# Six attention groups: scores times values and state products joined in one TensorE slot, ScalarE's steps in slots of their own

## The chip, the cores and the metric

One core of one Trainium2 chip runs the whole program. The metric is device time in microseconds from start to end of one execution, median of the runs. Engines are PE (TensorE; PEld is its weight load), DVE (VectorE), ACT (ScalarE), POOL (GpSimd) and SP (SyncE, which issues the DMAs).

## What is computed

The reference chains three parts, all in float32. Batch is 4, sequence 768.

```python
# attention with a decaying state, 8 heads of size 48
state = alpha[:, :, t, :, None] * state + einsum('bhd,bhe->bhde', k[:, :, t], v[:, :, t])
y[:, :, t] = einsum('bhd,bhde->bhe', q[:, :, t], state)
# x = y with its heads side by side: (4, 768, 384)
h = x.transpose(0, 2, 1) @ U @ V                 # token mixing of rank 32
u = x + h.transpose(0, 2, 1)
x = u + maximum(u @ w_ch1, 0) @ w_ch2            # 384 -> 1536 -> 384
h = maximum(x @ w_in, 0); u, v = halves(h)       # gated block, 384 -> 1024
x = (u * (w_spatial @ normed(v) + b_spatial)) @ w_out
```

## The kernel before

The attention of one batch is done in two groups of four heads. A group's sequence is cut into chunks of 128 positions. Inside a chunk the decayed scores are built in eight levels (steps 0 to 7); step 8 (`T_STEP`) transposes the keys, step 9 (`KV_STEP`) forms key-value products whose running sums are the states, steps 10 to 12 multiply scores with values (one for each of three PSUM banks `YB[y]`, L867), and step 13 (`Y_STEP`, L876) adds queries times states into the same three banks.

The attention of batch 0 runs first, alone. After it, a loop over the batches on every engine walks through a fixed list `UNITS1` of the first feed-forward's work: one token-mixing unit ("xu"), six transposing units ("u"), then 24 "h" units (`up`, L885) and 24 "z" units (`down`, L962 to L964), alternating with a lag of two. An "h" or "z" unit is nine matmuls of 128x384. Ahead of each unit every engine does the attention steps of batch b+1 that the table `SLOTS[b]` puts there. So for three batches, two groups each, six groups are woven in. A slot is the place ahead of one unit; a step's place in a group is `POSITION[n]`, a fraction of the group's half of the batch, and `step_slots` turns it into a unit by the units' estimated times. Engines follow their own instruction order and meet at semaphores only.

Which engine does what at a step (functions `att_step` on PE and ACT, `att_piece` on DVE):

- Steps 10 to 12: only PE works (the matmuls of L867, 32 for each step). `AV_STEP` is 10.
- Step 10 is also `START_STEP`: ACT copies the first two spreads of the next group's queries (L1045, four copies) with `att_start` and `att_second`, and DVE forms the next group's decay totals (L1338).
- Step 12 (`Y_STEP - 1`): ACT copies the states to `St` (L1138), two copies.
- Step 13: PE does L876 for all three banks, waiting for `state_ready` and for the last `q_ready`; ACT copies the three banks to `xn` (L1152); DVE scales the next group's queries (`PREFIX_STEP`, L1372 and L1374).

On PE step 10 waits for the copies of the scores (`a_act`, `ad_copied`), step 12 for the state sums of DVE (`state_step`), since its bank held the key-value products. With this table the four steps of a group have four slots in a row, between units that alternate "z", "h", "z", "h"; only in the first woven batch, second group, do steps 12 and 13 share one.

The two hidden-layer buffers of PSUM (`HB`) are emptied by ACT (L1190) and DVE (L1514): `up` of unit f waits for unit f-2's low parts, `down` of unit f for unit f's own, which is two "h" units back. SP's loads, the state sums of DVE and POOL's scaling (L655) are in the same order as the steps 0 to 9 need them. After the last batch's units the gated block runs by itself for all four batches.

Of the kernel before, what the change touches and what calls it, by code (L numbers as in the profile page):

```python
# [14 lines left out]
BATCH, HEADS, SEQ, HD = 4, 8, 768, 48  # L15
# [32 lines left out]
T_STEP, KV_STEP, AV_STEP = LEVELS, LEVELS + 1, LEVELS + 2  # L48
Y_STEP = AV_STEP + YB
STEPS = Y_STEP + 1  # L50

START_STEP, PREFIX_STEP = AV_STEP, Y_STEP
START, PREFIX = -1, -2


# [118 lines left out]
def step_slots(lead):  # L174

    ends = np.cumsum([time for _, _, time in UNITS1])
    slots = [[] for _ in UNITS1]
    for g in range(GROUPS):
        for n in range(STEPS):
            at = lead + (1 - lead) * (g + POSITION[n]) * SPREAD / GROUPS  # L180
            slots[int(np.searchsorted(ends, at * ends[-1]))].append((g, n))
    return slots


def vector_slots(slots):

    out, waiting = [], []
    for j, unit in enumerate(UNITS1):
        now = []
        for g, n in slots[j]:  # L190
            now += waiting
            waiting = [(g, n, piece) for piece in range(vector_pieces(n))]
            now += waiting
            waiting = []
            if n == START_STEP:
                now.append((g, START, 0))
            if n == PREFIX_STEP:
                now.append((g, PREFIX, 0))
        if not slots[j]:
            now += waiting[:1]  # L200
            waiting = waiting[1:]
        out.append(now)
    assert not waiting
    return out


def vector_pieces(n):

    return 2 if n < MASKED else NKV if n == KV_STEP else int(n < LEVELS)
# [1 line left out]


SPREAD = 0.96
POSITION = [(0.5 + 8.8 * n / KV_STEP) / 12 for n in range(AV_STEP)] + [x / 12 for x in (9.9, 10.4, 10.9, 11.4)]
ARENA = 212800
LEAD = [0.07] + [0.0] * (BATCH - 2)
SLOTS = [step_slots(lead) for lead in LEAD]
# [11 lines left out]
def build(nc, q, k, al, v, u_w, v_w, w1, w2, win, wst, wout, bias, ident_d, mask_d, out):  # L229
# [3 lines left out]
    with ExitStack() as ctx:  # L233
# [214 lines left out]
        def cut(src, hi, lo, n):  # L448
            flat = [x.rearrange("p a b -> p (a b)") for x in (src, hi[:, :, :], lo[:, :, :])]
            return [tuple(x[:, i * PIECE:(i + 1) * PIECE] for x in flat) for i in range(n)]  # L450

        first = cut(w1, w1h, w1l, W1_PIECES)
# [304 lines left out]
        def _(pe):  # L757
# [262 lines left out]
            for b in range(BATCH):  # L1020
                for j, (kind, i, _) in enumerate(UNITS1):
                    if b < BATCH - 1:
                        for g, n in SLOTS[b][j]:
                            att_step(b + 1, g, n, False)
                    if kind == "xu":
                        token_mix(b)
                    elif kind == "u":
                        mixed(b, i)
                    elif kind == "h":
                        up(b, i)  # L1030
                    else:
                        down(b, i)
# [7 lines left out]
        def _(act):  # L1040
# [53 lines left out]
            def att_step(a, g, n, first):  # L1094
                w = space(a, g)
                pa, pg = before(a, g)
                if 1 <= n < MASKED - 1:

                    act.wait_ge(q_ready[g], (LEVELS - 1) * a + n)
                    act.wait_ge(score_done[g], SCORES * a + n)  # L1100
                    spread(a, g, n + 1, False)
                if n == LEVELS - 2:

                    if first:
                        act.wait_ge(zeroed_a[g], 1)
                    else:

                        act.wait_ge(aux_done[pg], AUX * pa + AUX)
                    act.wait_ge(score_done[g], SCORES * a + n + 1)
                    L = block_size(n)  # L1110
                    for hh in range(2):
                        for m in range(2):
                            o = HALF * m + BLOCK * hh
                            bank = score_bank(w, n)[o:o + L, 0:UNITS * L].rearrange("p (u t) -> p u t", t=L)
                            dst = w.A[2 * L * m:2 * L * m + L, :, hh, 2 * L * m + L:2 * L * (m + 1)]
                            last = nc.scalar.copy(dst, bank)
                    last.then_inc(a_act[g], 1)
                if n == LEVELS - 1:

                    for p in range(PAIRS):  # L1120
                        act.wait_ge(score_done[g], SCORES * a + n + p + 1)
                        for hh in range(2):
                            bank = score_bank(w, n, p)[hh * HALF:(hh + 1) * HALF, 0:NCH * HALF]
                            last = nc.scalar.copy(w.A[0:HALF, p * NCH:(p + 1) * NCH, hh, HALF:CH],
                                                  bank.rearrange("p (u t) -> p u t", t=HALF))
                        last.then_inc(a_act[g], 1)
                if n == KV_STEP and not first:
                    square_copies(a, g, QUARTERS)
                if n == Y_STEP - 1:

                    if first:
                        act.wait_ge(zeroed_a[g], 2)
                    else:
                        act.wait_ge(aux_done[pg], AUX * pa + AUX)
                    act.wait_ge(state_step[g], NKV * (a + 1))
                    for hh in range(2):
                        r, e = slice(hh * ROW1, hh * ROW1 + HD), slice(hh * HD, (hh + 1) * HD)
                        last = nc.scalar.copy(w.St[r, :, :, e], w.Sc[r, :, :, :])  # L1138
                    last.then_inc(state_ready[g], 1)
                if n == T_STEP and not (first and g == 0):  # L1140
                    for x, units in enumerate(T_BANKS):
                        act.wait_ge(aux_done[g], AUX * a + x + 1)
                        nc.scalar.copy(w.kT[:, units[0]:units[-1] + 1, :],
                                       w.TB[x][:, 0:len(units) * ROWS].rearrange("p (u r) -> p u r", r=ROWS)
                                       ).then_inc(aux_act[g], 1)
                if n == Y_STEP:
                    if not first:

                        act.wait_ge(u_done, NU * a)
                    for y in range(YB):  # L1150
                        act.wait_ge(aux_done[g], AUX * a + AUX_KV + y + 1)
                        nc.scalar.copy(xn[:, 2 * y:2 * y + 2, g * GW:(g + 1) * GW],  # L1152
                                       w.YB[y][:, 0:2 * GW].rearrange("p (m x) -> p m x", m=2)
                                       ).then_inc(aux_act[g], 1)
# [115 lines left out]
            for b in range(BATCH - 1):  # L1270
                for j, (kind, i, _) in enumerate(UNITS1):
                    for g, n in SLOTS[b][j]:
                        att_step(b + 1, g, n, False)
                        if b == g == 0 and n in SPLITS2:
                            split_high(SPLITS2[n])
                        na, ng = after(b + 1, g)
                        if n == START_STEP and na < BATCH:
                            att_start(na, ng, False)
                            att_second(na, ng)
                    high(b, kind, i)  # L1280
                    if b == 0 and (kind, i) == ("u", NU - 1):
                        att_start(1, 0, False)
                        att_second(1, 0)
# [30 lines left out]
        def _(dve):  # L1314
# [354 lines left out]
            for b in range(BATCH):  # L1669
                for j, (kind, i, _) in enumerate(UNITS1):  # L1670
                    if b < BATCH - 1:
                        for g, n, piece in VECTOR_SLOTS[b][j]:
                            na, ng = after(b + 1, g)
                            if n == START and na < BATCH:
                                att_start(na, ng)
                            elif n == PREFIX and na < BATCH:
                                att_prefix(na, ng)
                            elif n >= 0:
                                if b == g == n == piece == 0:
                                    att_prefix(1, 0)  # L1680
                                att_piece(b + 1, g, n, piece, False)
                    low(b, kind, i)
                    if b == 0 and (kind, i) == ("u", NU - 1):
                        att_start(1, 0)
                    if b == BATCH - 1 and kind == "h" and i in COMBINES:
                        combine(COMBINES.index(i))
# [47 lines left out]
```

## Time and profile before

| what | us |
|---|---|
| median of 3 runs | 739.6 |
| lowest, highest run | 738.36, 743.63 |
| the profiled execution's own time | 741.86 |
| its span, first to last instruction | 740.1 |

The profile is of one execution. Each engine's row gives the time it was busy, its share of the span and its instructions. In a timeline a row is a run of like instructions in order: start, time to the end of the last, engine, line, tile written and read, count, and in brackets the idle time ahead and what ended it. Each matmul call of 32-bit floats of L867 and L876 appears as two MATMUL records, with two LDWEIGHTS records; the calls of L885 and L962 to L964 as one.

### The profile page before, as it was taken

How to read it: one execution, taken by the hardware profiler on the slowest of the kernel's cores; microseconds unless marked ns; L12 is line 12 of the kernel's file. 1: busy time of each engine (PE TensorE's matmuls, PEld its weight loads, DVE VectorE, ACT ScalarE, POOL GpSimd, SP SyncE). 2: the span in 40 equal slices, each digit the busy share in tenths (PEclk: the TensorE clock that was granted, in tenths of full speed). 3: DMA queues.
4: the chain of work that ended last, by engine and by line, in shares of the span. 5: the costliest groups of instructions: out<-in, count | busy, mean ns of one | idle time of the engine just before them, and what ended most of it. 6: DMA issues, size and time to landing. Idle time of an engine off the chain costs nothing.

```text
span 740.1 us, 25675 instructions
## 1 busy us (share of the span) xinstructions
PE 703.6 (95%) x11336; PEld 664.0 (90%) x11336; DVE 395.9 (53%) x668; ACT 338.4 (46%) x573; POOL 210.5 (28%) x141
## 2 busy tenths in 40 slices
PE   2798899999999999999999999999999999999998
PEld 2688789899998899999999899999998998999998
DVE  6888674544664555555553324225933851870671
ACT  5787546435546346446435331334433432532422
POOL 5504480320350220161120231462360060033022
PEclk9999999999999999999999999999999999999999
DMA  9414501211401221311000251002110101101001
GB/s 360 157 46 148 176 4 45 99 57 45 152 4 45 73 83 45 118 37 45 22 18 2 91 150 72 33 11 87 64 40 26 65 12 53 64 0 64 0 0 64
DMA packets 16525, 49.49 MB, mean 67 GB/s; under 512 B 1616, under 2 KB 9552, under 8 KB 15920
## 3 DMA queue, kind: packets, MB, share of 16 engines
q1 hardware_dynamic: 16432, 48.09, 18.5%
q8 instruction: 77, 1.26, 0.7%
q14 instruction: 16, 0.13, 0.1%
HBM read 38.65 MB, written 9.44 MB: 65 GB/s over the span
## 4 chain that ended last, share of the span: by engine, by line
PE 67%; issue 19%; POOL 4%; DVE 3%; ACT 1%; DMA 0%; POOLq 0%; DVEq 0%; ACTq 0%
PE HB L885 23%; PE ZB L962 7%; PE ZB L964 7%; PE ZB L963 7%; PE SB L762 4%; PE ZB L885 3%; PE SB L885 3%; POOL gl L712 3%; PE SB L867 2%; PE SB L876 2%; PE SB L822 2%; POOL x2l L686 1%; PE SB L999 1%; PE SB L837 1%; PE SB L850 1%
## 5 line engine op out<-in xcount | busy, mean ns | idle before, releaser
L1514 DVE SCALAR_TENSOR_TENSOR hid_lo<-HB,hid_hi 128x384 fp32r<-128x384 f32 x96 | 53.3, 556 | 140.9 <-ACT hid_hi L1190 140.1
L1190 ACT ACTIVATE hid_hi<-HB 128x384 fp32r<-128x384 f32 x96 | 47.2, 492 | 158.9 <-PE HB L885 158.7
L885 PE MATMUL HB<-uh,w1h 128*128 128x384 f32 x288 | 103.0, 358 | 4.1 <-DVE ul L1510 1.5
L962 PE MATMUL ZB<-hid_hi,w2h 128*128 128x384 f32 x288 | 98.6, 342 | 0.0
L885 PE MATMUL HB<-ul,w1h 128*128 128x384 f32 x288 | 96.7, 336 | 0.0
L964 PE MATMUL ZB<-hid_lo,w2h 128*128 128x384 f32 x288 | 96.6, 335 | 0.0
L885 PE MATMUL HB<-uh,w1l 128*128 128x384 f32 x288 | 96.5, 335 | 0.0
L963 PE MATMUL ZB<-hid_hi,w2l 128*128 128x384 f32 x288 | 96.3, 334 | 0.0
L1045 ACT COPY Qd<-Q 48x768 f32<-48x768 f32 x84 | 73.0, 870 | 13.6 <-PE SB L762 5.0
L712 POOL TENSOR_TENSOR gl<-gf,gh 128x384 fp32r<-128x384 f32 x32 | 33.2, 1044 | 147.8 <-ACT gh L1230 147.4
L655 POOL TENSOR_TENSOR Q<-Q,bk 112x768 f32<-112x768 f32 x13 | 24.7, 1902 | 174.4 <-ACT Qd L1045 174.4
L762 PEld LDWEIGHTS SB<-Qd,K 112*32 112x32 f32 x4032 | 42.1, 116 | 25.4 <-issue 16.8
L762 PE MATMUL SB<-Qd,K 112*32 112x32 f32 x4032 | 46.9, 205 | 16.1 <-DMA K<-in_k 9.3
L655 POOL TENSOR_TENSOR Q<-Q,small 112x768 f32<-112x768 f32 x26 | 42.0, 1617 | 67.8 <-PE SB L810 31.3
L885 PEld LDWEIGHTS HB<-uh,w1h 128*128 128x128 f32 x288 | 54.0, 187 | 6.6 <-issue 1.4
L1331 DVE TENSOR_TENSOR K<-K,small 112x768 f32<-112x768 f32 x26 | 47.7, 1834 | 16.8 <-PE SB L822 9.5
L1606 DVE BATCH_NORM_STATS2 stats<-vf 128x6 f32<-128x512 f32 x24 | 16.5, 692 | 73.1 <-ACT vf L1234 73.1
L885 PEld LDWEIGHTS HB<-uh,w1l 128*128 128x128 f32 x288 | 54.2, 188 | 1.3 <-issue 1.3
L962 PEld LDWEIGHTS ZB<-hid_hi,w2h 128*128 128x128 f32 x288 | 54.0, 188 | 1.1
L885 PEld LDWEIGHTS HB<-ul,w1h 128*128 128x128 f32 x288 | 54.0, 188 | 0.2 <-issue 0.2
L963 PEld LDWEIGHTS ZB<-hid_hi,w2l 128*128 128x128 f32 x288 | 54.1, 188 | 0.0
L964 PEld LDWEIGHTS ZB<-hid_lo,w2h 128*128 128x128 f32 x288 | 54.1, 188 | 0.0
(260 smaller groups left out, 1516.4 us busy)
## 6 DMA issues: line engine op xcount, KB each, us to landing
Q<-in_q SPq DMA_DIRECT2D x8, 768.0 KB, 6.0
AL<-in_al SPq DMA_DIRECT2D x7, 768.0 KB, 4.9
K<-in_k SPq DMA_DIRECT2D x7, 768.0 KB, 4.3
Vt<-in_v SPq DMA_DIRECT2D x8, 576.0 KB, 3.9
mid<-x2s SPq DMA_DIRECT2D x8, 576.0 KB, 3.6
x<-mid SPq DMA_DIRECT2D x4, 1152.0 KB, 5.3
out<-o_sb SPq DMA_DIRECT2D x24, 192.0 KB, 1.8
x2s<-in_w SPq DMA_DIRECT2D x9, 384.0 KB, 4.6
```

The costliest lines, as they stand in the source:

```text
L655: nc.gpsimd.tensor_tensor(qq, qq, t.broadcast_to([ROWS, FLAT // (2 * L), L]), ALU.mult).then_inc(q_ready[g], 1)
L712: nc.gpsimd.tensor_tensor(gl[:, f, t], gf[:, f, t], gh[:, f, t].bitcast(F32), ALU.subtract).then_inc(gl_done, 1)
L762: last = nc.tensor.matmul(bank[j * BLOCK:(j + 1) * BLOCK, u * BLOCK:(u + 1) * BLOCK], keys[:, first_key:first_key + BLOCK], queries[:, u, ...
L885: last = nc.tensor.matmul(dst, weights(x, w), moving(y, m), start=(n == 0 and x == y == 0), stop=(n == total - 1 and y == 1))
L962: nc.tensor.matmul(bank, w2h[:, i, cols], hi, start=(i == 0), stop=False)
L963: nc.tensor.matmul(bank, w2l[:, i, cols], hi, start=False, stop=False)
L964: nc.tensor.matmul(bank, w2h[:, i, cols], lo, start=False, stop=(i == F1B - 1)).then_inc(z_done, 1)
L1045: nc.scalar.copy(space(a, g).Qd[0 if first else n % 2][r, :, hh, :].rearrange("p u (n l) -> p u n l", l=block_size(n)), targets(Q[g][r, :] ...
L1190: nc.scalar.activation(hid_hi[:, i % HID, :], HB[i % 2][:, 0:TILE], ACT.Relu).then_inc(h_hi, 1)
L1331: nc.vector.tensor_tensor(kk, kk, t.broadcast_to([ROWS, FLAT // (2 * L), L]), ALU.mult).then_inc(k_ready[g], 1)
L1514: nc.vector.scalar_tensor_tensor(hid_lo[:, i % HID, :], HB[i % 2][:, 0:TILE], 0.0, hid_hi[:, i % HID, :].bitcast(F32), ALU.max, ALU.subtra ...
L1606: nc.vector.bn_stats(stats[:, i, :], vf[:, i, :]).then_inc(stat_done, 1)
```

## The change

The table of positions gets two more entries, numbers 14 and 15, that are no steps of PE or DVE but slots for ACT: `SPREADS_SLOT` at 9.9/12, where step 10 stood, and `STATES_SLOT` at 10.8/12, near where step 12 stood. Steps 10 to 13 all go to 11.3/12, which is the unit where step 13 stood. Steps are now put into slots in order of position. PE skips numbers 14 and 15.

By the table, steps 10, 11 and 12 of a group move from units 24, 25 and 26 to unit 27, and from 48, 49 and 50 to 51 (first woven batch: from 26, 27, 28 to 29, and from 49, 50 to 51). The order of instructions on DVE, POOL and SP is the same as before; on ACT too, except that in the first woven batch the second group's state copies come one unit earlier. Batch 0's attention is not touched.

```diff
-START_STEP, PREFIX_STEP = AV_STEP, Y_STEP
+PREFIX_STEP = Y_STEP
+SPREADS_SLOT, STATES_SLOT = STEPS, STEPS + 1
...
     for g in range(GROUPS):
-        for n in range(STEPS):
+        for n in sorted(range(len(POSITION)), key=lambda n: POSITION[n]):
             at = lead + (1 - lead) * (g + POSITION[n]) * SPREAD / GROUPS
...
-            if n == START_STEP:
+            if n == SPREADS_SLOT:
                 now.append((g, START, 0))
...
-POSITION = [(0.5 + 8.8 * n / KV_STEP) / 12 for n in range(AV_STEP)] + [x / 12 for x in (9.9, 10.4, 10.9, 11.4)]
+POSITION = [(0.5 + 8.8 * n / KV_STEP) / 12 for n in range(AV_STEP)] + [x / 12 for x in (11.3, 11.3, 11.3, 11.3, 9.9, 10.8)]
...
                         for g, n in SLOTS[b][j]:
-                            att_step(b + 1, g, n, False)
+                            if n < STEPS:
+                                att_step(b + 1, g, n, False)
...
-                if n == Y_STEP - 1:
+                if n == (Y_STEP - 1 if first else STATES_SLOT):
...
-                        if n == START_STEP and na < BATCH:
+                        if n == SPREADS_SLOT and na < BATCH:
                             att_start(na, ng, False)
                             att_second(na, ng)
...
-                            elif n >= 0:
+                            elif 0 <= n < STEPS:
```

## Rows read from the trace of the kernel before

**Rows 1.** Page: busy time of each engine; the chain that ended last, by engine
```profile
PE 703.6 (95%) x11336; PEld 664.0 (90%) x11336; DVE 395.9 (53%) x668; ACT 338.4 (46%) x573; POOL 210.5 (28%) x141
...
PE 67%; issue 19%; POOL 4%; DVE 3%; ACT 1%; DMA 0%; POOLq 0%; DVEq 0%; ACTq 0%
```

**Rows 2.** Timeline of PE, one group's steps 10 to 13 in their four slots
```profile
229.03 0.33 PE L885 MATMUL HB<-uh,w1l 128*128 128x384 f32 x1
229.20 0.34 PE L885 MATMUL HB<-ul,w1h 128*128 128x384 f32 x1
229.47 0.89 PE L867 MATMUL SB<-Vt,A 128*32 128x48 f32 x64
230.28 0.44 PE L962 MATMUL ZB<-hid_hi,w2h 128*128 128x384 f32 x1
230.56 0.33 PE L963 MATMUL ZB<-hid_hi,w2l 128*128 128x384 f32 x1
...
232.07 0.72 PE L867 MATMUL SB<-Vt,A 128*32 128x48 f32 x48
233.09 0.38 PE L867 MATMUL SB<-Vt,A 128*32 128x48 f32 x16 [0.30 <-issue]
233.39 0.44 PE L885 MATMUL HB<-uh,w1h 128*128 128x384 f32 x1
...
237.51 0.34 PE L964 MATMUL ZB<-hid_lo,w2h 128*128 128x384 f32 x1
237.78 1.86 PE L876 MATMUL SB<-St,Q 112*32 112x96 f32 x80
239.57 0.44 PE L885 MATMUL HB<-uh,w1h 128*128 128x384 f32 x1
239.85 0.34 PE L885 MATMUL HB<-uh,w1l 128*128 128x384 f32 x1
```

**Rows 3.** Timeline of PE, the group whose steps 12 and 13 share a slot
```profile
176.51 0.34 PE L964 MATMUL ZB<-hid_lo,w2h 128*128 128x384 f32 x1
176.77 0.89 PE L867 MATMUL SB<-Vt,A 128*32 128x48 f32 x64
177.48 1.84 PE L876 MATMUL SB<-St,Q 112*32 112x96 f32 x80
179.25 0.45 PE L885 MATMUL HB<-uh,w1h 128*128 128x384 f32 x1
179.54 0.34 PE L885 MATMUL HB<-uh,w1l 128*128 128x384 f32 x1
```

**Rows 4.** Timeline of ACT beside the slots of rows 2
```profile
230.09 3.70 ACT L1045 COPY Qd<-Q 48x768 f32<-48x768 f32 x4
235.29 0.49 ACT L1190 ACTIVATE hid_hi<-HB 128x384 fp32r<-128x384 f32 x1 [1.50 <-PE HB L885]
235.80 1.20 ACT L1138 COPY St<-Sc 48x480 f32<-48x480 f32 x2
```

**Rows 5.** DMA queue q8 and busy times, 90 to 411; busy times between two stalls
```profile
q8 instruction: 57, 0.93, 1.2%
...
90.00:411.00 321.00, 316.98 (x7216) 292.97 (x7215) 170.45 (x279) 161.69 (x273) 85.42 (x55) 1.00 0.15 52
...
192.27:233.07 40.80, 40.50 (x885) 37.41 (x885) 23.29 (x38) 22.55 (x37) 18.47 (x12) 1.00 0.17 57
```

**Rows 6.** A stall of PE; queue q8 in windows 149.1:150.2 and 152.8:153.9
```profile
150.30 0.56 PE L762 MATMUL SB<-Qd,K 112*32 112x32 f32 x41
151.52 0.47 PE L762 MATMUL SB<-Qd,K 112*32 112x32 f32 x34 [0.65 <-issue]
...
q8 instruction: 1, 0.02, 5.8%
...
q8 instruction: 1, 0.02, 5.5%
```

**Rows 7.** Busy times of the shortest 256 instructions of PE without a stall
```profile
92.81:95.73 2.92, 2.92 (x131) 2.63 (x134) 2.01 (x3) 2.81 (x4) 2.44 (x2) 1.00 0.03 8
```

## The prediction

> **What bounds the kernel now.** I read the page first: PE is busy for 703.6 of 740.1 us, DVE and ACT for about half of it, and the chain that ended last lies on PE and on its own issue for 86% [rows 1]. From 90 to 411 us, where the six woven groups run, PE is busy for 316.98 of 321.00 us [rows 5]. So in this stretch time is what PE's instruction order costs: what another engine does counts only where PE comes to wait for it. The second view is the timeline of PE around one group's steps 10 to 13 [rows 2]. It shows three things: how long a slot of small matmuls keeps the large ones away, that there is extra time at both of its edges, and one gap of PE inside a slot that no other engine ended ("issue"). The third view, queue q8, says what that gap is [rows 5, 6].
>
> **The switches that go.** Large matmuls start 0.17 us apart (229.03, 229.20) [rows 2]. The slot of step 10 lies between the starts 229.20 and 230.56: 1.36 us, less the two steps of 0.17 that would be there anyhow, is 1.01. Inside it 64 records start in 0.89 - 0.21 = 0.68 us, 10.8 ns apart (0.21 is the last record's own length, 233.09 to 233.47 less its 15 steps), so about 0.33 us of the slot is no matmul at all: 0.10 us on entering, 0.13 us after the last one, 0.10 us after the first large one. Step 13 alone takes 239.85 - 237.51 - 0.35 = 1.99 us [rows 2]. Where steps 12 and 13 share a slot, both take 179.54 - 176.51 - 0.35 = 2.68 us [rows 3]. Separate they cost 1.01 + 1.99 = 3.00, so one slot fewer saves 0.32 us. This is the kernel's own example of the change, and I take its price. Five groups have four slots each, which become one (three fewer each, 15); the group that already shares one loses two. 17 x 0.32 = 5.4 us saved. For the unseen join of step 10 to 11 the bounds are 0.29 (all but a quarter change of 0.05) and 0.33 us, which moves the sum by 0.3 at most.
>
> **What the joined slot adds: instruction fetch.** Every matmul is two instructions here, weights and product. PE ran 14431 of them from 90 to 411, and queue q8 moved 57 packets, 0.93 MB, in that time [rows 5]: one packet of 16 KB for each 253 recorded instructions, 256 with those of registers and semaphores that are not counted. The same number stands between stalls: from the one ending at 192.27 to the one ending at 233.07 PE and PEld have 885 + 885 = 1770 instructions, 1792 = 7 x 256 with 22 uncounted ones [rows 5]. So PE's stream comes in pages of 256, and such gaps stand on page borders. How late a page can be is seen at 150.30 to 151.52 [rows 6]. PE stops in the middle of a run of step 3's matmuls; the only q8 packet near starts and ends within 149.1 to 150.2 and takes 5.8% of 16 x 1.1 us, 1.0 us; PE goes on at 151.52, at least 1.3 and about 1.4 us after it landed. The next packet lies within 152.8 to 153.9, so it started 1.3 us after PE had entered the new page. I read this as: the next page is asked for on entering the present one, and can be run 1.3 + 1.0 + 1.4 = 3.7 us later. Before, that is nearly always hidden, since between two slots of small matmuls lie 9 or 18 large ones at 0.17 us.
>
> The joined slot is 3 x 64 + 80 = 272 products, 544 instructions, on end. Wherever it starts, it holds one whole page. A page of step 10 to 12 matmuls alone lasts 128 x 10.8 ns = 1.4 us; one that is half step 13 (80 records in 1.86 - 0.25 = 1.6 us, 20 ns each) lasts 2.0. Counting on from the border at 233.09 (which assumes that the stream's length ahead of each group stays), borders fall 9, 62, 188, 205, 76 and 93 instructions into the six slots, so four slots hold a page of the short sort and two a mixed one (196 and 179 instructions of it short, 1.7 us): 1.5 us as a mean. PE's sequencer runs ahead of the array by a queue that no row shows; I give it 0.6 us, and its bounds are 0 and 1. The stall is then 3.7 - 1.5 - 0.6 = 1.6 us in each group, 6 x 1.6 = 9.6 us. Bounds: 256 instructions passed without a stall in 2.92 us [rows 7], so the wait may be as short as that: 2.9 - 1.5 = 1.4, 8.4 us in all. From below nothing excludes zero, if that page was only luckily placed and more than one is held ready. From above, a page can come later than 3.7: the page ahead of the stall of rows 6 held 18 large matmuls (3.1 us) and parts of two slots, some 4.4 us of work, and PE still waited. Stalls of twice the size, 3.1 us, would give 18.6. I take 9.6, nearest to the one fetch that the rows show whole.
>
> The 0.5 us stall ahead of 233.09 (48 records take 0.72 with the last one's 0.21, so the next was due at 232.59) [rows 2] sits in a slot that goes; stalls of that sort will fall elsewhere by chance, and half of it, 0.2, is counted as gained, which rounding swallows.
>
> The Trainium skill, page "Runtime: NRT & Kernel Launch", section "Instruction fetch mechanics", says that instructions come in blocks of 16 KiB (256), the next one while the present is run, which the 57 packets bear out. The same section gives PE's buffer as 2048 instructions and says that issue is slower than the filling, so that a border's cost is mostly hidden; by that no stall would come in 544 instructions, and the sum would be -5.4 alone. The gap at 151.52 speaks against it.
>
> **The cover that goes.** ACT's four spreads (3.70 us from 230.09) ran beside the slots of steps 10 and 11, and its state copies (1.20 us) beside step 12 [rows 4]. Now large matmuls alone lie beside them. With unit "h" 9 ending at time 0 (229.47), PE does a "z", an "h" and a "z" unit, 9 x 0.173 = 1.56 us each, and enters the joined slot at 4.7. ACT is done with the spreads at 4.3, with the next hidden half (0.49) at 4.8 and with the states at 6.0; step 13 can start at 4.7 + 0.3 + 2.1 = 7.1 without any stall. "z" unit 10, which needs that hidden half, comes only after the joined slot. So 1.1 us stay over and I cost the moves on ACT at nothing. Step 12's wait for the state sums was met before the first slot, and DVE's, POOL's and SP's order stays; the K load of the next group is issued ahead of these slots. After the joined slot the copies to `xn` come at the same place as before. If the spreads began over 1.1 us late, step 13 would pay the rest.
>
> **Sum.** Against the profiled execution, 741.9 (span 740.1 and 1.8 around it): -5.4 + 9.6 - 0.2 = +4.0, so 745.9. That execution stands 2.3 us above the median of 739.6; for the median I forecast 739.6 + 4.0 = 743.6, rounded to 743.5. A measurement of this kernel can tell about 1% (7.4 us) from no change, so this is no change that can be told, on the slow side.
>
> **Rivals.**
> - Fetch keeps up (a second page is held ready, or the queue's lead covers the rest): only the switches count, 739.6 - 5.4 = 734. For it: a shared slot of 144 products had no stall [rows 3], and a page in 2.92 us had none [rows 7]. Against it: 144 products need not hold a whole page, and the stalls at 151.52 and 233.09 are there [rows 2, 6]. Chance 0.25.
> - Late fetches decide, the case that is clearly slower: the packet in a joined slot starts late, as the one in rows 6 must have, because other transfers or pages stand before it, and some slots pay twice (the first group's third border falls inside its slot). Each group then pays about 3 us: 18 - 5 = +13, 752. It decides from 2.2 us a stall upward (13 less 5.4 is over 7.4 us). For it: the page of rows 6 was such a fetch. Against it: no load of SP is issued near the joined slots. Chance 0.12.
> - The lost cover: the spreads or state copies finish late and step 13 waits for `state_ready`. Their 1.2 us behind the hidden half, in all six groups, would cost up to 7 us beside the -5.4: 741. The margin of 1.1 us speaks against it [rows 4], and in a stall it is hidden. Chance 0.08.
>
> **How the numbers follow.** The forecast has 0.55. Its own range is 740 to 747 (stalls of 1.0 to 2.1 us). Leaving out half of the late case and the edge of the first, the range is 733.5 to 749. Faster by over 1% (under 732.2) needs more than all switches, 0.05; slower by over 1% (over 747.0) is the late case and a little of the forecast's upper end, 0.14; within 1% is the rest, 0.81.
>
> **What would show it.** Right: one slot a group on PE with 192 records of L867 and 80 of L876, at 10.8 and 20 ns, and in each a gap of 1 to 2 us ended by "issue", a q8 packet landing about 1.4 us before its end; idle time of PE by issue up by some 9 us; step 13 never ended by ACT. Wrong: joined slots of about 4.0 us without a gap (0.3 + 2.1 + 1.6), which is the first rival; gaps ended by ACT L1138, which is the third; or a slot pace slower than 10.8 ns because the sequencer cannot feed 544 instructions so quickly, which no row here excludes beyond 144 products.

## The result and the profile after

| | median | lowest to highest |
|---|---|---|
| before, runs beside | 738.98 us | 738.21 to 743.63 |
| changed | 745.08 us | 743.03 to 745.44 |
| ratio, 95% interval | 1.0068 | 1.0043 to 1.0093 |

The changed kernel is 0.7% slower, clear of no change by its interval, and less than the 1% that the chances were drawn at. The forecast was 743.5 us. In microseconds the ratio is 5.0 of 739 (3.2 to 6.9); the two medians lie 6.1 apart, inside that interval.

The page of the changed kernel hardly shows where the time went. PE is busy for less time over a longer span, with the same number of instructions as in rows 1:

```profile
span 741.2 us, 25675 instructions
PE 696.9 (94%) x11336; PEld 662.1 (89%) x11336; DVE 395.5 (53%) x668; ACT 338.3 (46%) x573; POOL 210.6 (28%) x141
```

The waits of PE from 90 to 416 us (engine, tile and line, what ended the idle time: total, times, longest) name the place. L868 and L877 are what L867 and L876 were:

```profile
PE SB L868 <- issue: 5.3, 3, 1.9
PE SB L877 <- issue: 3.7, 3, 1.4
PE SB L763 <- issue: 0.9, 2, 0.6
PE SB L823 <- issue: 0.4, 1, 0.4
```

Six idle times, one for each woven group, none ended by another engine. The timeline of PE at the third group's joined slot, which answers to rows 2:

```profile
233.71 0.34 PE L965 MATMUL ZB<-hid_lo,w2h 128*128 128x384 f32 x1
233.98 2.25 PE L868 MATMUL SB<-Vt,A 128*32 128x48 f32 x192
236.04 0.84 PE L877 MATMUL SB<-St,Q 112*32 112x96 f32 x29
237.98 1.35 PE L877 MATMUL SB<-St,Q 112*32 112x96 f32 x51 [1.09 <-issue]
239.25 0.44 PE L886 MATMUL HB<-uh,w1h 128*128 128x384 f32 x1
239.53 0.34 PE L886 MATMUL HB<-uh,w1l 128*128 128x384 f32 x1
```

192 products run at the old pace, 10.8 ns each (2.25 less the last one's 0.2), then step 13 breaks off after its 29th product, 221 products or 442 instructions into the slot. The forecast put a page border 188 instructions in, and the next 256 later, at 444. In the second group, which answers to rows 3, the break is in the middle of L868:

```profile
173.37 1.90 PE L868 MATMUL SB<-Vt,A 128*32 128x48 f32 x158
176.93 0.55 PE L868 MATMUL SB<-Vt,A 128*32 128x48 f32 x33 [1.66 <-issue]
```

158 products are 316 instructions; the forecast's border was at 62 + 256 = 318. Ahead of this break queue q8, which loads instructions, moves one packet in the window 174.3:175.5 and none from 175.5 to 178:

```profile
q8 instruction: 1, 0.02, 4.9%
```

4.9% of 16 x 1.2 us is 0.9 us. The packet has landed by 175.5, and PE goes on 1.4 us later, at 176.93. The next table sets all six breaks beside the forecast. A slot's time is from the start of the large matmul ahead to that of the second one after, less the two steps of 0.17 (for the third group 239.53 - 233.71 - 0.35 = 5.47; by unrounded starts 5.48); without a stall it is 4.05 (see the first experiment).

| group | forecast: border inside at instruction | break seen after products (x 2) | slot, us | stall, us |
|---|---|---|---|---|
| 1 | 265, 521 | 260 (520) | 5.77 | 1.7 |
| 2 | 318 | 158 (316) | 5.93 | 1.9 |
| 3 | 444 | 221 (442) | 5.48 | 1.4 |
| 4 | 461 | 230 (460) | 5.60 | 1.5 |
| 5 | 332 | 166 (332) | 6.05 | 2.0 |
| 6 | 349 | 174 (348) | 6.14 | 2.1 |

The slots together take 34.96 us. The 23 slots of the kernel before took 30.46, the 0.5 us stall ahead of 233.09 in it. That is +4.5 us, +5.0 without that stall.

Counted through the whole trace, with the semaphore and register instructions that the timelines leave out, all six breaks stand 100 or 101 instructions past a multiple of 256. So do the gaps of the kernel before at 151.52, 233.09 and 258.22.

One border of the forecast passed without a gap: that at instruction 265 of the first group, though the page ahead of it held only short products, 1.4 us of work. Its packet lies in the window 118:119.4, ahead of the joined slot, which starts at 120.33:

```profile
q8 instruction: 1, 0.02, 4.2%
```

So it was asked for well before PE itself reached the border at instruction 9 (120.36). PE's sequencer was ahead there, among the large matmuls: by about 3.3 us, if a packet is asked for 1.1 to 1.2 us before it starts (that is how long after the breaks of groups 2 to 6 the next packet starts). In the other five slots, where the earlier border lies among small products, the packet starts 0.6 to 1.0 us after PE has passed that border, so the sequencer was ahead by 0.2 to 0.6 us only. These are estimates from the packets' times.

ACT's cover holds, as forecast. The timeline of ACT at the third group, beside rows 4:

```profile
229.92 3.64 ACT L1047 COPY Qd<-Q 48x768 f32<-48x768 f32 x4
233.58 0.49 ACT L1192 ACTIVATE hid_hi<-HB 128x384 fp32r<-128x384 f32 x1
234.10 1.20 ACT L1140 COPY St<-Sc 48x480 f32<-48x480 f32 x2
```

The states are ready at 235.30, and step 13 starts at 236.04 on its own time. The margin is 0.7 us, where the forecast had 1.1.

### The profile page after: what moved, and what is told of

It reads as the page before. It is cut to its first block, busy times and chain, and to the rows that moved or that the text cites. A ratio compares the mean times of both kernels' runs of the same rounds, so it can differ in the third digit from the quotient of the medians.

```text
span 741.2 us, 25675 instructions
## 1 busy us (share of the span) xinstructions
PE 696.9 (94%) x11336; PEld 662.1 (89%) x11336; DVE 395.5 (53%) x668; ACT 338.3 (46%) x573; POOL 210.6 (28%) x141
## 4 chain that ended last, share of the span: by engine, by line
PE 65%; issue 20%; POOL 4%; DVE 4%; ACT 1%; DMA 0%; POOLq 0%; DVEq 0%; ACTq 0%
PE HB L886 23%; PE ZB L963 7%; PE ZB L965 7%; PE ZB L964 7%; PE SB L763 4%; PE ZB L886 3%; PE SB L886 3%; POOL gl L713 3%; PE SB L868 2%; PE SB L877 2%; POOL x2l L687 1%; PE SB L823 1%; PE SB L1000 1%; PE SB L851 1%; DVE K L1333 1%
```

## The experiments

**Two pairs.** Steps 10 and 11 share a slot, 12 and 13 another, 18 large matmuls apart (9 in the second group).

```diff
-POSITION = ... [x / 12 for x in (11.3, 11.3, 11.3, 11.3, 9.9, 10.8)]
+POSITION = ... [x / 12 for x in (10.4, 10.4, 11.3, 11.3, 9.9, 10.8)]
```

> Steps 10 and 11 share one slot, steps 12 and 13 another, 18 large matmuls apart; ACT's slots stay as in the changed kernel. Theory (a slot saves 0.32 us for each switch that goes, and a stall comes only where a slot holds a whole page of 256 instructions): 11 switches go, 3.6 us; a slot has 256 or 288 instructions, so at most one group has a stall, 0.2 us in all. Time about 3.5 us under the kernel before (735.5), ratio 0.995, and some 9 us under the changed one less the 6 switches it keeps: 7.5 us under it. Rival (the time went to something else in the joining, such as lost cover of ACT's copies or waits for the states): the loss stays in part, ratio 0.998 to 1.005. No gap of PE over 0.3 us by issue inside these slots under the theory.

Measured: 734.87 us (734.27 to 736.84) beside 739.61, ratio 0.9941 (0.9921 to 0.9961). It is faster than both kernels (the interval is that against the kernel before). The timeline of PE in the third group:

```profile
227.82 0.34 PE L965 MATMUL ZB<-hid_lo,w2h 128*128 128x384 f32 x1
228.09 1.57 PE L868 MATMUL SB<-Vt,A 128*32 128x48 f32 x128
229.59 0.44 PE L886 MATMUL HB<-uh,w1h 128*128 128x384 f32 x1
229.87 0.33 PE L886 MATMUL HB<-uh,w1l 128*128 128x384 f32 x1
...
232.66 0.34 PE L965 MATMUL ZB<-hid_lo,w2h 128*128 128x384 f32 x1
232.93 0.89 PE L868 MATMUL SB<-Vt,A 128*32 128x48 f32 x64
233.63 1.84 PE L877 MATMUL SB<-St,Q 112*32 112x96 f32 x80
235.41 0.45 PE L886 MATMUL HB<-uh,w1h 128*128 128x384 f32 x1
235.69 0.34 PE L886 MATMUL HB<-uh,w1l 128*128 128x384 f32 x1
```

The joint of two steps of 64 products takes 229.87 - 227.82 - 0.35 = 1.70 us where two slots took 2.04, so a switch is worth 0.34 there; the second slot takes 2.68, as in rows 3. None of the twelve slots has an idle time by issue in the list of waits; the second slots of the first and second group take 2.84 and 2.79 us, 0.1 to 0.15 more. Together the twelve take 26.56 us, 3.4 less than the 29.96 of before without its stall, where 3.6 was expected. Put together, the four steps without a stall take 1.70 + 2.68 less one more switch, 4.05 us: this is the estimate of what the joined slot would have taken. So joining does no harm by itself; what harms is a run of short instructions without large matmuls in between.

**Three and one.** Which groups stall is decided by where the borders fall.

```diff
-POSITION = ... [x / 12 for x in (11.3, 11.3, 11.3, 11.3, 9.9, 10.8)]
+POSITION = ... [x / 12 for x in (10.9, 10.9, 10.9, 11.3, 9.9, 10.8)]
```

> Steps 10 to 12 share a slot (384 instructions), step 13 stands alone one unit later, except in the second group of the first woven batch, where all four are joined. Theory: which groups stall depends on where the page borders fall. Counting on, the second, fifth and sixth group hold a whole page and stall for 1.9 us each; in the first the border stands so early that the sequencer's lead over the large matmuls covers nearly all (0 to 0.6); the third and fourth have none. 12 switches go, 3.9 us, stalls 5.6 us: time within 2 us of the kernel before or slightly over. Rival (any slot over some length stalls, by the length alone): all six groups alike, either all near 1.5 us or none.

Measured: 742.07 us (738.79 to 745.98) beside 739.61, ratio 1.0027 (1.0000 to 1.0053). Stalls of 1.8, 1.9 and 2.3 us stand in the second, fifth and sixth group, as expected, and in no other slot of 192 products (the second group's is the one with all four steps). The first group, where 0 to 0.6 was expected, has none. The fourth group, without, and the fifth, with one (timeline of PE):

```profile
285.96 2.25 PE L868 MATMUL SB<-Vt,A 128*32 128x48 f32 x192
...
344.55 2.07 PE L868 MATMUL SB<-Vt,A 128*32 128x48 f32 x175
348.28 0.40 PE L868 MATMUL SB<-Vt,A 128*32 128x48 f32 x17 [1.66 <-issue]
```

The same 192 products with the same neighbours run through in one group and break in another. A rule that goes by a slot's length alone falls with that. Step 13's own slots, 9 large matmuls after, took 1.99 us in the first, fourth and fifth group, but 2.41 in the third and 2.67 in the sixth. In the third a page border lies inside step 13, and weight loads stop there for 0.3 us. In the sixth it is the clock: it follows the 2.3 us stall.

```profile
404.80:408.90 4.10, 4.10 (x46) 3.60 (x49) 0.00 (x0) 0.09 (x1) 0.00 (x0) 0.58 0.01 4
```

The granted clock is 0.58 as a mean here, so mostly its lower level, 1.2 GHz, and in between large matmuls start 0.32 us apart in place of 0.17. Both add to the forecast of +1.7 us (stalls 5.6 less switches 3.9); by the medians it is +2.5.

**Sixty-four more instructions.** The borders are moved, nothing else.

```diff
             for g, n in LAST_STEPS:
                 att_step(0, g, n, True)
+            for _ in range(64):
+                pe.sem_inc(passed, 1)
```

> The changed kernel with 64 more semaphore instructions on PE ahead of the first woven batch; nothing else differs. Theory: the borders stay at every 256 instructions of the stream, so in each joined slot they come 64 instructions (32 products) earlier, and the stall moves with them or jumps to the next border: in products from the slot's start (gap ahead of it) from about 159 to 255 in the second group, 222 to 190 in the third, 230 to 198 in the fourth, 166 to 262 in the fifth, 174 to 270 in the sixth, 260 to 228 in the first. Stalls 8.9 us in all against 10 in the changed kernel. Rival (the stall comes after a fixed number of instructions in a slot, since the sequencer can't feed them so quickly, or with a PSUM bank): the places stay where they are.

Measured, one run with a profile (749.47 us; the 64 instructions run before the woven part, where they cost several us themselves, so the time is not read): the breaks come after 228, 254, 190, 198, 261 and 270 products; 228, 255, 190, 198, 262 and 270 were expected. In the second group (timeline of PE) the break has gone from the 158th product to the 254th:

```profile
181.41 2.25 PE L868 MATMUL SB<-Vt,A 128*32 128x48 f32 x192
183.47 1.51 PE L877 MATMUL SB<-St,Q 112*32 112x96 f32 x62
185.69 0.68 PE L877 MATMUL SB<-St,Q 112*32 112x96 f32 x18 [0.71 <-issue]
```

The stalls make 34.46 - 6 x 4.05 = 10.2 us in all; I had expected 8.9. So the stall belongs to a place in PE's instruction stream, every 256 instructions, and not to a step, a bank or a time in the slot.

**ACT without slots of its own.** This undoes the part of the change that keeps ACT's work apart.

```diff
-POSITION = ... [x / 12 for x in (11.3, 11.3, 11.3, 11.3, 9.9, 10.8)]
+POSITION = ... [x / 12 for x in (11.3, 11.3, 11.3, 11.3, 11.28, 11.29)]
```

> The changed kernel without slots of their own for ACT: the next group's spreads and the state copies come in the joined slot's unit. Theory: ACT begins them after the hidden half of the last h unit and has the states ready about 8.6 us after the h unit of my count, where step 13 is due at 7.1; in the three groups whose fetch stall lies ahead of step 13 (second, fifth, sixth) that costs nothing, in the other three up to 1.5 us each, part of it beside their own stall: 0 to 3 us over the changed kernel, 745 to 748. Rival (ACT's cover mattered much in the change): over 5 us above the changed kernel, with step 13 ended by ACT's state copies in all six groups.

Measured: 748.63 us (745.52 to 752.03) beside 739.61, ratio 1.0127 (1.0087 to 1.0167), against 1.0068 of the changed kernel. Step 13 waits for ACT in the three groups named and in no other. The timelines of PE and of ACT in the third group, and the granted clock (the fraction behind the busy times, 1.00 or 0.68) right after its wait, ahead of it, and right after the fourth group's wait:

```profile
236.21 2.25 PE L868 MATMUL SB<-Vt,A 128*32 128x48 f32 x192
240.40 2.61 PE L877 MATMUL SB<-St,Q 112*32 112x96 f32 x80 [1.94 <-ACT St L1140]
```
```profile
235.27 3.77 ACT L1047 COPY Qd<-Q 48x768 f32<-48x768 f32 x4
239.06 1.19 ACT L1140 COPY St<-Sc 48x480 f32<-48x480 f32 x2
```
```profile
240.40:243.00 2.60, 2.60 (x81) 2.32 (x81) 0.50 (x1) 0.96 (x2) 0.00 (x0) 0.68 0.02 6
230.00:236.00 6.00, 6.00 (x36) 5.96 (x35) 3.22 (x13) 2.84 (x5) 0.00 (x0) 1.00 0.01 3
297.76:299.70 1.94, 1.94 (x81) 1.79 (x82) 0.51 (x1) 0.98 (x3) 0.00 (x0) 1.00 0.05 8
```

ACT's order forces it: spreads and states come only after the last "h" unit's hidden half. In these three groups PE's wait takes the place of the fetch stall, since the next page arrives meanwhile. The six slots take 38.69 us, 3.7 more than in the changed kernel. I had 0 to 3. Some 2.0 us of it is a lower clock: right after the waits of the first and third group the granted clock is 0.65 and 0.68 over 2.6 us, and step 13 takes 2.72 and 2.61 in place of 1.86; these slots take 7.20 and 7.14 us. After the fourth group's wait of the same 1.94 us the clock stays at 1.00, and the slot takes 6.18. The rival's six waits did not come, but the cost is real: slots of their own for ACT are needed by the join.

**The ACT slots alone.** The other part of the change, with PE's steps where they stood before.

```diff
-POSITION = ... [x / 12 for x in (11.3, 11.3, 11.3, 11.3, 9.9, 10.8)]
+POSITION = ... [x / 12 for x in (9.9, 10.4, 10.9, 11.4, 9.9, 10.8)]
```

> The other half of the change alone: ACT's spreads and state copies at positions of their own (9.9 and 10.8), PE's steps 10 to 13 where they stood before. Only the second group of the first woven batch gets its state copies one unit earlier. Theory (the whole difference comes from joining PE's steps): the time of the kernel before, ratio 0.997 to 1.003. Rival (part of the loss is ACT's new order): the ratio of the changed kernel in part, 1.003 or more.

Measured: 739.36 us beside 739.19, ratio 0.9991 (0.9976 to 1.0006). The interval is -1.8 to +0.4 us, and the 23 slots take 29.96 us, as before without the stall. So, within that, the loss of the changed kernel comes from PE's join.

**Nine between.** How much large work between two pairs is enough.

```diff
-POSITION = ... [x / 12 for x in (11.3, 11.3, 11.3, 11.3, 9.9, 10.8)]
+POSITION = ... [x / 12 for x in (10.9, 10.9, 11.3, 11.3, 9.9, 10.8)]
```

> Two pairs as in the first experiment (10 with 11, 12 with 13), but with only 9 large matmuls (1.56 us) between the pairs instead of 18; in the second group of the first woven batch all four steps are joined. Theory (a page must last about 3.7 us less the sequencer's lead): the joined group stalls 1.9 us, the others hardly at all (a page with one pair's half, 9 large matmuls and the other's half lasts about 3 us: 0 to 0.4 us each). 12 switches go, 3.9 us, stalls about 2.3 us: 1 to 2 us under the kernel before. Rival (the refill after a border needs more work than that): stalls of 0.5 us and more in all five two-slot groups.

Measured: 738.12 us (735.54 to 741.79) beside 739.19, ratio 0.9982 (0.9961 to 1.0003): not told from no change, though 1.1 us under, within what was expected. The one joined group stalls (slot 6.20 us, gap after 158 products), of the five others two by 0.3 and 0.5 us. The rival (0.5 us and more in all five) did not come; nine large matmuls between two pairs are just about enough here, eighteen are enough.

**Half the instructions.** The same work in outputs of 64 rows.

```diff
-                            for t in HALVES if first else QUARTERS:
+                            for t in HALVES:
...
-                            for t in (WHOLE if first else QUARTERS) if c else []:
+                            for t in (WHOLE if first else HALVES) if c else []:
```

> The changed kernel with the outputs of steps 10 to 13 cut in halves of 64 rows instead of quarters of 32: the same arithmetic with half the instructions, 96 + 40 products, 272 instructions a slot. Theory (pages of instructions): a slot hardly ever holds a whole page, so there is no gap by issue over 0.3 us, although the matmuls themselves last longer (29 ns each for step 10 to 12 by batch 0's part, so 2.8 us in place of 2.1, and some 2.0 for step 13): a slot of about 5.1 us in place of 5.8 us, 4 us under the changed kernel. Rival (the stall goes by the time or the length of the joined work): the gap stays and the time rises by what the slower matmuls cost, some 6 us over the changed kernel.

Measured: 738.32 us (737.38 to 740.98) beside 739.19, ratio 0.9985 (0.9969 to 1.0002). Its six slots take 28.83 us, 6.1 less than the changed kernel's 34.96, and the two ratios are 6.1 us apart too; I had expected 4. The timeline of PE in the third group:

```profile
233.07 3.00 PE L868 MATMUL SB<-Vt,A 128*64 128x48 f32 x96
235.90 1.84 PE L877 MATMUL SB<-St,Q 112*64 112x96 f32 x40
```

All six slots take 4.80 us without an idle time, though scores times values are slower (3.00 against 2.25). Step 13 is no slower than in quarters (1.84 against 1.86), which I had at 2.0; that, times six, is part of the surplus. The matmuls themselves took longer and the stall went: what counts is how many instructions fall on each microsecond of them.

**The fetch by itself.** Scores times values three times over.

```diff
-                    for m, p, c, u, o0 in output_blocks(y):
+                    for rep, (m, p, c, u, o0) in [(r, x) for r in range(1 if first else 3) for x in output_blocks(y)]:
...
-                                                        start=(m == p == hh == 0), stop=False, skip_group_check=True)
+                                                        start=(rep == m == p == hh == 0), stop=False,
+                                                        skip_group_check=True)
```

> The fetch measured by itself: the changed kernel with every product of scores times values of the woven groups done three times (so these attention outputs count that term threefold). A joined slot then holds 576 + 80 products, 1312 instructions, five pages' worth. Theory (the next page is asked for on entering the present one and can be run 3.7 us later): inside a slot PE stops at every border, and the starts after two such stops in a row lie 256 instructions and 3.7 us apart (3.4 to 4.1), where 128 products take 1.4 us; 4 or 5 stops a slot, each gap 2.3 us, the first one of a slot shorter by the sequencer's lead. One instruction packet of queue q8 starts about 1.3 us after each start. Slots of 16 to 18 us in place of 8.2. Rival (more than one page is held ready, and the stall of the changed kernel is a start-up cost of a long run): one gap a slot, and a pace of 10.8 ns after it.

Measured, one run with a profile (819.19 us beside 739.82). The timeline of PE in the first group, and queue q8 in the windows 132:133.2 and 135.7:137:

```profile
125.95 3.00 PE L868 MATMUL SB<-Vt,A 128*32 128x48 f32 x260
130.96 1.57 PE L868 MATMUL SB<-Vt,A 128*32 128x48 f32 x128 [2.02 <-issue]
134.69 1.57 PE L868 MATMUL SB<-Vt,A 128*32 128x48 f32 x128 [2.16 <-issue]
138.42 0.83 PE L868 MATMUL SB<-Vt,A 128*32 128x48 f32 x58 [2.16 <-issue]
```
```profile
q8 instruction: 1, 0.02, 5.7%
...
q8 instruction: 1, 0.02, 5.6%
```

Runs of exactly 128 products begin 3.73 us apart (130.96, 134.69, 138.42), where 128 products take 1.4. Each q8 packet lies in a window that opens 1.0 us after such a start: 5.7% of 16 x 1.2 us is 1.1 us, so it has landed by 133.2, and PE goes on 1.5 us later. One page at a time, 3.7 us each: the gap is no start-up cost. The other groups give 3.4 to 4.0 us from start to start, 3.2 once for the first page of a slot. There are 3 or 4 stops a slot (4 or 5 expected): the first group passes its border at instruction 265 without one, as in the changed kernel. Slots take 16.3 to 18.8 us (16 to 18 expected). The clock does not set this pace. In the fourth group it is at its lower level, 1.2 GHz, for a whole page:

```profile
340.01:343.74 3.73, 2.79 (x128) 2.61 (x128) 0.00 (x0) 0.00 (x0) 0.00 (x0) 0.50 0.02 4
```

The 128 products then take 2.79 us in place of 1.57, the next gap shrinks to 0.95, and the starts are 3.73 us apart all the same.

## Why the prediction was right, step by step

- *The switches that go.* Forecast 0.32 us each, 17 of them, 5.4 us. By unrounded starts rows 3 give 0.33, and the joint of two equal steps (1.70 us for 2.04) gives 0.34; the slots before without their stall, 29.96 us, less six of the estimated 4.05 is 5.7 us. Right, 0.3 short.
- *The fetch stall.* Forecast 1.6 us in each group, 9.6 in all. Measured 34.96 - 6 x 4.05 = 10.7 us, 1.4 to 2.1 a group. The mechanism, the place of each break and the 3.7 us were right. The term that was undersized is the stall of a page of short products (forecast 1.7, seen 1.9 to 2.1 in groups 2, 5, 6), because the 0.6 us given for the sequencer's lead was too much: 3.7 - 1.4 - 2.0 leaves 0.3. The forecast had said that no row showed this lead.
- *The first group* came out at 1.7 us by luck. The forecast counted it among the slots with one page of short products. It holds two whole pages, from instruction 9 to 265 and from 265 to 521. The first, of short products, cost nothing, because its successor was asked for among the large matmuls; the stall belongs to the second, of 60 short products and 68 of step 13, about 2.0 us of work. A lead fixed in microseconds cannot give this; it is long among large matmuls and short among small ones.
- *The lost cover* at nothing: right, and shown from both sides. With ACT's slots alone nothing changes, without them step 13 waits in three groups. The margin was 0.7 us and not 1.1: step 13 came 2.06 us after the slot's start, not 0.3 + 2.1.
- *The sum.* Forecast +4.0 us; the slots give +5.0 without the old stall, and the ratio +5.0 (3.2 to 6.9). The two terms were short by 0.3 and 1.1 us in opposite directions, so their errors cancel in part.
- *The base.* The profiled execution of before stood 2.3 us above its median. It was treated as an offset that both kernels carry. It holds chance stalls outside the slots that changed (the 0.65 us of rows 6 is one, another of 1.4 us ends at 258.22), 3.3 us in all from 90 to 411; in the changed kernel's profile the idle times by issue outside the joined slots are only 1.3 us in the list of waits above. That is 2.0 of the 3.4 us by which the slots (+4.5) exceed the difference of the two spans (+1.1); the other 1.4 us were not traced. The changed kernel's profiled execution, 743.03 us, is also 2.1 us under its own median, so the two profiled executions are no measure of the difference.
- *The rival that fetch keeps up* fell with the six breaks. That two pairs come near its number, 734.87 against 734, is in part chance: two pairs drop 11 of the 17 switches, which is 3.4 us by the slots, and the median is 4.7 us under. The rival of late fetches did not come: the largest stall was 2.1 us, under the 2.2 from which it was to decide.

What stays open: why some packets start later than 1.1 to 1.3 us after PE has gone on at a border (the chance stalls of before; after the first group's break in the changed kernel it is 2.0 us), and how many instructions the sequencer's lead is. No run was made for either.

## What to carry to other kernels

Joining short matmuls to save switches pays about a third of a microsecond a switch, but the joined run should not hold a whole page of 256 instructions, weight loads counted, unless that page lasts nearly 4 us. (One such page passed here, because it began right behind large matmuls.) So count instructions for each microsecond of PE before joining: 128 small products in 1.4 us starve in the middle of a run, the same work in pairs with 18 large matmuls between does not, nor does it with larger tiles and half the instructions. An idle time that ends by "issue" in the middle of one line's run, at a multiple of 256 instructions from the next such one, is the sign of it, and it can be told from the trace of the kernel before.

## What the runs showed of the hardware beyond what was expected

- PE does not get ahead of its fetches at this pace: with pages of 1.4 us of work, the pages inside a slot took 3.4 to 4.0 us from start to start (3.2 once), and 3.73 where the clock was at its lower level. The Trainium skill, page "Runtime: NRT & Kernel Launch", section "Instruction fetch mechanics", has the block of 256 instructions right; its 2048 instructions for PE and its mostly hidden border do not fit these six breaks, and the measurement decides.
- Entering or leaving a run of small tiles among full-size matmuls costs 0.33 us for both edges. The Trainium skill, page "TensorEngine Tiling (Array Packing)", section "Key Properties", says that changing the tiling mode drains TensorE; it gives no figure. The rows show extra time at both edges, and not what passes in it.
- After idle times of nearly the same length TensorE's clock fell in some cases and not in others. Without slots for ACT it was 0.65 and 0.68 after waits of 1.89 and 1.94 us and 1.00 after another of 1.94; with three and one it was 0.58 after an idle time of 2.08 us; with nine between it stayed at 1.00 after 1.93. The changed kernel's six breaks (idle up to 1.86 us) left the mean at 1.000 in its profile; in one of its other three runs it was 0.998. So what decides is not shown.
- Outputs of 64 rows in place of 32 made step 13 no slower (1.84 us for 40 products, 1.86 for 80), while scores times values took 3.00 in place of 2.25.
